# First layer of three experts by seven block products over even and odd tiles

## The reference

```python
def _moe_ref(x, domain_probs, w1, w2):          # x 1536x320, w1 4x320x1024, w2 4x1024x320
    p = domain_probs / (domain_probs.sum(-1, keepdims=True) + 1e-09)
    out = np.zeros((N, D), dtype=np.float32)
    for e in range(E):
        h = np.maximum(x @ w1[e], 0.0)
        out += p[:, e:e + 1] * (h @ w2[e])
    return out.astype(np.float32)
# the recurrence, for every token t:
#   C = f*C + i*outer(v, k);  n = f*n + i*k;  y = sigmoid(o) * (C @ q) / max(|n.q|, 1)
```

## Time and profile before

| what | value |
|---|---|
| median of 3 executions | 417.52 us |
| the profiled execution's own time | 416.59 us |
| its span, first to last instruction | 414.9 us |
| PE busy | 409.5 us (99%), 2698 matmuls |
| DVE, ACT, POOL busy | 180.0, 158.7, 147.4 us |
| granted TensorE clock | 0.999 of full speed |

### The profile page before, as it was taken

How to read it: one execution, slowest core, us unless ns; L and a number is a source line. 1 busy time by engine, 2 the same in 40 slices (tenths; PEclk the granted TensorE clock), 3 DMA queues, 4 the chain that set the end, 5 groups by cost and what they waited for, 6 DMA issues and landing times.

```text
span 414.9 us, 7006 instructions
## 1 busy us (share of the span) xinstructions
PE 409.5 (99%) x2698; PEld 396.1 (95%) x2698; DVE 180.0 (43%) x370; ACT 158.7 (38%) x329; POOL 147.4 (36%) x183
## 2 busy tenths in 40 slices
PE   8999999999999999999999999999999999999997
PEld 8889999999999999999999999999999999999996
DVE  6875796746555556446223232313123232311323
ACT  5475477745355643524122431234111342211111
POOL 5855735594175935302001650075100453000000
PEclk9999999999999999999999999999999999999999
DMA  8899939678513835300000331024200000000101
GB/s 276 268 294 377 355 106 362 233 261 284 190 43 118 311 124 206 125 2 0 2 0 2 92 125 63 0 71 140 71 0 0 2 0 2 34 0 0 65 0 65
DMA packets 16899, 48.45 MB, mean 117 GB/s; under 512 B 1921, under 2 KB 8594, under 8 KB 15714
## 3 DMA queue, kind: packets, MB, share of 16 engines
q1 hardware_dynamic: 16290, 46.60, 32.6%
q10 hardware_dynamic: 576, 1.40, 1.0%
HBM read 45.94 MB, written 2.05 MB: 116 GB/s over the span
## 4 chain that ended last, share of the span: by engine, by line
PE 96%; DVE 1%; ACT 1%; issue 1%; POOL 0%; DVEq 0%; POOLq 0%; ACTq 0%
PE hid_ps L1077 41%; PE acc_ps L1096 36%; PE out_ps L1033 5%; PE score_ps L1096 3%; PE out_ps L1040 2%; PE acc_ps L1077 2%; PE score_ps L977 2%; PE hid_ps L926 1%; PE add_ps L1012 1%; PE score_ps L972 1%; ACT dec_w L553 1%; PE acc_ps L1033 0%; PE out_ps L1052 0%; PE out_ps L1054 0%; PE out_ps L1053 0%
## 5 line engine op out<-in xcount | busy, mean ns | idle before, releaser
L811 DVE SCALAR_TENSOR_TENSOR h_lo<-hid_ps,h_hi 128x384 fp32r<-128x384 f32 (+2 forms) x120 | 68.0, 566 | 218.5 <-ACT h_hi L588 218.4
L588 ACT ACTIVATE h_hi<-hid_ps 128x384 fp32r<-128x384 f32 (+2 forms) x120 | 59.8, 498 | 230.7 <-PE hid_ps L1077 230.6
L1096 PE MATMUL acc_ps<-w_hi,h_hi 128*128 128x320 f32 x352 | 110.2, 313 | 0.0
L1096 PE MATMUL acc_ps<-w_hi,h_lo 128*128 128x320 f32 x352 | 108.8, 309 | 0.0
L1096 PE MATMUL acc_ps<-w_lo,h_hi 128*128 128x320 f32 x352 | 108.4, 308 | 0.0
L441 POOL TENSOR_TENSOR w_lo<-w_raw,w_hi 128x384 fp32r<-128x384 f32 x56 | 58.8, 1052 | 130.0 <-ACT w_hi L574 130.0
L1077 PE MATMUL hid_ps<-xt_hi,w_lo 128*128 128x384 f32 (+2 forms) x360 | 103.8, 342 | 0.6 <-POOL w_lo L441 0.6
L1077 PE MATMUL hid_ps<-xt_hi,w_hi 128*128 128x384 f32 (+2 forms) x360 | 104.2, 344 | 0.1
L1077 PEld LDWEIGHTS hid_ps<-xt_hi,w_lo 128*128 128x128 f32 x360 | 65.4, 188 | 5.0 <-POOL w_lo L441 0.8
L1096 PEld LDWEIGHTS acc_ps<-w_lo,h_hi 128*128 128x128 f32 x352 | 66.3, 188 | 1.3
L1096 PEld LDWEIGHTS acc_ps<-w_hi,h_hi 128*128 128x128 f32 x352 | 66.3, 188 | 1.3
...
## 6 DMA issues: line engine op xcount, KB each, us to landing
...
```

Of the source, the lines that this page charges most:

```text
L588: nc.scalar.activation(h_hi[:, M % RING, 0:cols], hid_bank(M)[:, 0:cols], ACT.Relu).then_inc(hid_hi, 1)
L811: nc.vector.scalar_tensor_tensor(h_lo[:, M % RING, 0:cols], hid_bank(M)[:, 0:cols], 0.0, h_hi[:, M % RING, 0:cols].bitcast(fp32), ALU.max, ...
L1096: last = nc.tensor.matmul(acc_ps[t][:, 0:DM], x, w, start=(f == 0 and i == 0), stop=(f == NF - 1 and i == 2))
```

## The change

Three experts on the later tiles are taken out of the slots: expert 2 on tiles 6 to 11, experts 1 and 0 on tiles 4 to 11. Ten groups (80 slots) are left, and expert 0 is loaded twice. The work taken out becomes 12 *steps*. A step takes two hidden blocks at a time and pairs of an even and an odd tile (3 pairs for expert 2, 4 pairs for the others). The first layer of a step is a product of a 2 x 2 block matrix of weights (2 hidden blocks by 2 halves of the 320 input rows, 160 each) and a 2 x 2 block matrix of `x` (2 halves of rows by even and odd tiles). It is computed with seven block products rather than eight, in the order 1, 6, 5, 7, 2, 4, 3. A product is 4 matmuls of pairs x 128 columns (128 rows high x high, low x high, high x low, and one over 96 rows with the three parts of the other 32).

The operands are sums. `t_hi`, `t_lo` and `rest` (sums and differences of `x`) are made once, in slots 64 to 72. For that, 24 DMAs copy 32-row pieces of `xt_hi` to other partitions (`load_rest`). The sums of the weights are made in each step: GpSimd makes the four sums (`step_sums`) and residuals (`own_lows`, `step_down_low`), ScalarE rounds (`own_highs`, `sums_highs`, `step_down_high`), VectorE makes residuals (`sums_lows`, `step_rest_low`). After the products VectorE, ScalarE and GpSimd combine them (`add_2`, `add_3`, `add_21`, `add_12`, `keep_1`, `keep_5`, `add_22`), then come ReLU and residual for each of the four blocks (`wide_relu`, `wide_low`). The second layer stays as it was: `wide_down`, 6 matmuls of 320 columns for one tile and two hidden blocks. The products of step 0 stand in slots 73 to 79, one at the end of each.

The core of the diff:

```diff
-LOADS = (0, 1, 2, 3, 2, 1, 0)
-GROUPS = ((0, 0, 2), (1, 0, 2), (1, 2, 2), (2, 0, 3), (2, 3, 3), (3, 0, 3), (3, 3, 3), (3, 6, 3), (3, 9, 3),
-          (4, 6, 3), (4, 9, 3), (5, 4, 4), (5, 8, 4), (6, 10, 2), (6, 2, 4), (6, 6, 4))
+LOADS = (0, 1, 0, 2, 3)
+GROUPS = ((0, 0, 2), (1, 0, 2), (1, 2, 2), (2, 2, 2), (3, 0, 3), (3, 3, 3), (4, 0, 3), (4, 3, 3), (4, 6, 3), (4, 9, 3))
-T0 = {2: 2, 3: 6, 4: 16, 5: 22, 6: 28, 7: 32, 8: 38, 9: 44, 10: 48, 11: 54}
+T0 = {2: 2, 3: 6, 4: 16, 5: 22, 6: 30, 7: 35, 8: 41, 9: 47, 10: 51, 11: 57}
+EXPERTS = (2, 1, 0)
+FIRST_PAIR = (1, 0, 0)
+ORDER = (1, 6, 5, 7, 2, 4, 3)
+BEGIN = 73
# SyncE
+            def load_rest():
+                wait_attention(sp)
+                for part, raised, lowered in ((rest_hi, 64, 96), (rest_lo, 0, 32)):
+                    for k, first in enumerate((raised, lowered)):
+                        source = halves(xt_hi[first:first + 32, 2, :].bitcast(fp32))
+                        for r in range(3):
+                            for half in range(2):
+                                to = part[32 * r:32 * (r + 1), (0, 3, 1, 2)[2 * k + half], :]
+                                sp.dma_start(to.rearrange(...), source[:, half, :, :]).then_inc(rest_in, 16)
...
+                if M == T0[NT - 1] + 7:
+                    load_rest()
# GpSimd
+            def rest_whole(first):
+                pool.wait_ge(rest_in, 24 * 16)
+                both = rest_hi[:, first:first + 2, :]
+                nc.gpsimd.tensor_tensor(both, both, rest_lo[:, first:first + 2, :], ALU.add).then_inc(rest_ready, 1)
...
+            for t in range(1, STEPS):
+                if t + 1 < STEPS:
+                    step_sums(t + 1)
+                    own_lows(t + 1)
+                    step_down_low(t + 1)
+                add_22(t)
# ScalarE, at the end of slots 68 and 71
+                if M == 68:
+                    round_rest(0, 3)          # waits for both rest_whole
...
+                if M == 71:
+                    round_rest(3, 2)          # waits for the four sums of turn_rest
+                    round_rest(5, 2)
# VectorE, a step
+            for t in range(1, STEPS):
+                add_wide(t, 0)
+                add_2(t)
+                add_wide(t, 1)
+                add_wide(t, 2)
+                add_3(t)
+                add_wide(t, 3)
+                if t + 1 < STEPS:
+                    sums_lows(t + 1)
+                wide_low(t, 11)
+                add_21(t)
+                if t + 1 < STEPS:
+                    step_rest_low(t + 1)
+                wide_low(t, 22)
+                wide_low(t, 21)
+                add_12(t)
+                wide_low(t, 12)
# TensorE
+                nc.tensor.matmul(to, hi[:, 0:128], x_hi, start=m in (1, 5, 6), stop=False, skip_group_check=True)
+                nc.tensor.matmul(to, lo, x_hi, start=False, stop=False, skip_group_check=True)
+                nc.tensor.matmul(to, hi[:, 0:128], x_lo, start=False, stop=False, skip_group_check=True)
+                nc.tensor.matmul(to, hi[0:REM, 128:256], rest[:, right, cols(t)], start=False, stop=True, ...)
...
+                if M >= BEGIN:
+                    product(0, ORDER[M - BEGIN])
+            for t in range(1, STEPS + 2):
+                ahead, behind = halves_of(t)
+                turns = [(half_of, i) for half_of in (ahead, behind) if half_of is not None for i in range(pairs(half_of[1]))]
+                for n in range(8):
+                    if t < STEPS and n < len(ORDER):
+                        product(t, ORDER[n])
+                    at = n if t > 1 else n - 1
+                    if 0 <= at < len(turns):
+                        wide_down(*turns[at][0], turns[at][1])
```

More of the change, by code:

```diff
@@ L123, with pair_of, pairs, downs_done @@
 LAST_GROUP = {n: max(a for a, g in enumerate(GROUPS) if g[1] <= n < g[1] + g[2]) for n in range(NT)}
+CLASSIC = EVICT[-1][0] + GROUPS[-1][2]
+def pair_of(t):
+    return FIRST_PAIR[2 * t // NF]
+def pairs(t):
+    return PAIRS - pair_of(t)
+def downs_done(t):
+    return sum(pairs(p) for p in range(t + 1))
+def wide_evictions(p, half, i):
+    before = [pairs(2 * b) for b in range(p // 2) for _ in range(2)] + [pairs(p)] * half
+    return CLASSIC + sum(before) + i + 1
+def last_evictions():
+    out = []
+    for pair in range(PAIRS):
+        p = max(p for p in range(1, STEPS, 2) if pair_of(p) <= pair)
+        out += [(wide_evictions(p, half, pair - pair_of(p)), FIRST_WIDE + 2 * pair + half) for half in range(2)]
+    return out
+def bank_freed(p, half, i):
+    if half == 1:
+        return wide_evictions(p, 0, i)
+    return wide_evictions(p - 2, 1, min(i, pairs(p - 2) - 1))
+def product_count(t, m):
+    return len(ORDER) * t + ORDER.index(m) + 1
+def halves_of(t):
+    first, second = ((0, t - 1), (1, t - 2)) if t % 2 == 0 else ((1, t - 2), (0, t - 1))
+    return [(half, p) if 0 <= p < STEPS else None for half, p in (first, second)]
 def wait_if(eng, sem, count):
@@ new lines, in build @@
+        x_nat = first("x_nat", [L, B, DM])
+        apart = raw[:, :, :, :, :].rearrange("p k t h l -> p k (t h l)")
+        attention.close()
+        t_hi, t_lo, rest = sb("t_hi", [128, 4, WIDE], f32r), sb("t_lo", [128, 4, WIDE], f32r), sb("rest", [REM, 7, WIDE], f32r)
+        left_hi, left_lo = sb("left_hi", [128, 2, 7, 256], f32r), sb("left_lo", [128, 2, 7, 128], f32r)
+        whole = between("whole", [128, 4, WIDE])
+        rest_hi, rest_lo = between("rest_hi", [REM, 4, WIDE]), between("rest_lo", [REM, 4, WIDE])
@@ L1195 @@
         "w_b": w.reshape(NE, NF // 2, 2, 128, WB).transpose(0, 1, 3, 2, 4),
+        "w_s": steps.reshape(STEPS, 128, SUM_AT),
     }
```

441 lines of the change are left out of this document (408 added, 33 removed).

## The result

| | before | after |
|---|---|---|
| time, median of 4 runs each (lowest to highest) | 417.39 us (416.86 to 417.92) | 429.14 us (427.77 to 430.61) |
| ratio | | 1.028, 95% interval 1.024 to 1.032 |
| profiled execution, time and span | 416.59, 414.9 | 430.01, 428.3 |

The change made the kernel 2.8% slower, 11.8 us between the medians. The forecast was slower too, but by 2.6 to 3 us, and 429 lies outside its range of 410 to 425.5.

A forecast was written before the change was run, and what follows sets the result against it. PE was taken as the bound, its time proportional to streamed columns plus waits. -10.1 + 5.9 + 7.2 = +3.0 us on 416.59 gave 419.6, or 420.5 by the median; forecast 420, range 410 to 425.5.

The forecast's parts named there:

- What it removes: On PE, 16 matmuls of 384 columns and 32 of 512 go: 10.1 us less.
- Slots 0 to 63: Before slot 64, same kind of work per slot on each engine: priced at nothing, 0 to 1 us.
- Part 1: Slots 64 to 73, operands from x: 24 DMA issues take 9.3 us; PE waits 1.7 us if nothing interferes.
- Part 2: Slots 67 to 73: VectorE and GpSimd exclude each other, raising PE's waits to 5.9 us instead of 1.7.
- a sign of being wrong: Forecast is wrong if L1279 and L1288 on VectorE keep to 0.65 and 1.07 us.
- Part 3: Steps 1 to 5: PE waits on VectorE's chains, 4.5 us without meeting GpSimd, 7.2 us with it.
- Part 4: Steps 6 to 11: VectorE needs 4.2 us against PE's 4.5, so nothing waits, by 0.3 us.
- rival (c): Steps 6 to 11 wait too, at each first wide_down on block 21's residual: 6 us more, 426; chance 0.12.
- the bound of 427: Upper end of the unknown: the longest VectorE and GpSimd operations in every encounter give about 427 us.

The follow-up runs named there:

- Experiment 5: Changed kernel with VectorE's two subtractions of unit 6's rounded scores in slots 25 and 26 in place of 26 and 28; 427.26 us, ratio 1.025.
- experiment 10: On top of experiment 9: the next step's own blocks rounded and their residuals formed earlier, tile-sum evictions ahead of x's gate in slots 39 and 55; 416.30 us, 0.996.
- experiment 8: Changed kernel with the 24 transfers of load_rest read from DRAM (rows of the weights) instead of xt_hi in SBUF; 426.71 us, ratio 1.023.
- Experiment 1: Changed kernel with 12 DMAs in load_rest instead of 24, each carrying both halves in the tiles' own order; 424.50 us, ratio 1.016.
- experiment 6: On top of Experiment 1 and Experiment 5: GpSimd forms one rest-row sum, VectorE the other and turn_rest's four subtractions, ScalarE's round_rest placed where its input is ready; 421.78 us.
- experiment 9: On top of experiment 6: VectorE forms both rest-row sums, GpSimd's step_sums(1) moves from slot 70 to 64, t_lows(0) and rest_lows(0, 3, 0) one slot later; 421.46 us.
- Experiment 11: Changed kernel with GpSimd's sums and residuals of the weights of steps 2 to 11 on 16, 8 and 32 columns only; 426.12 us, ratio 1.022.
- experiment 2: Changed kernel with 42 unused matmuls of 384 columns put ahead of block 70's second layer; 430.12 us, ratio 1.030.
- experiment 3: Changed kernel with DN_END 24 in place of 28, so GpSimd, not VectorE, takes the second-layer weight residuals of blocks 24 to 27; 430.78 us, ratio 1.031.
- experiment 4: Changed kernel with step_rest_low on one of seven weight blocks (128 columns in place of 896); 425.19 us, ratio 1.019.
- experiment 12: On top of experiment 10: step_rest_low(0), t_lows(0), rest_lows(0, 3, 0), own_highs(0) and sums_highs(0) in earlier slots, own_highs(1) one later; 411.75 us, ratio 0.986.

## Why the prediction was wrong

**What it removes: right.** -10.2 us measured for -10.1, and a step of seven products with four pairs takes 13.5 us where 13.4 was forecast. The 0.229 us per 512 columns of the earlier trace rows held after the change as well. The Trainium skill's 131 ns for them (TensorE: Matmul & The Clock Gate, section Back-to-back issue gap) did not show up here either.

**Slots 0 to 63: the first failed step.** "I price that at nothing" (0 to 1 us) measured +6.3 us. The argument was that each engine has the same kind of work per slot. It has, but in 2-tile slots, which are shorter, and with unit 6's subtractions at other slots relative to it. The order shows it: VectorE's second `subtract_high` of unit 6 now stands behind `xt_low(5)`, before the change it stood ahead of it, and the scores that need it fall in the slot without a block ahead. I had not followed this part of the order. Experiment 5 shows that this one place makes PE's wait of 2.1 us, and with it the low clock that can follow. The waits of 0.6 us at 135 and 192 us are two evictions that stand behind x's gate; in experiment 10, which puts them ahead of it, 0.3 us remain of each, before scores.

**Part 1, the issue of 24 transfers: the second failed step.** "Three take 1.16 us, so 24 take 9.3 us" measured 16.0. The earlier trace rows were transfers from DRAM; these read SBUF, and by experiment 8 that is 0.60 against 0.43 us an issue. It shifted the chain by 6.6 us, and 7.2 us of wait appeared in one piece before block 70 in place of 1. Experiment 1 takes the issue back to 8.8 us and gives 5.0 us of waits, with 5.9 forecast. Of the 9.9 us of the changed kernel 7.2 are this wait and 2.7 low clock. The other links (2.4, 1.5, 0.49 and 0.56 us) held to a tenth.

**Part 2, the meetings: right as a mechanism, absent in the changed kernel's own stretch.** Operations of 0.69 us took 2.8 beside GpSimd's in experiments 1 and 6, and 0.69 once it was idle (experiment 9). In the changed kernel GpSimd began only when VectorE had already run dry: `sums_lows` (L1279) took 0.69 and `step_rest_low` (L1288) 1.08 there, which the prediction had named as a sign of being wrong. The rule in the Trainium skill (SBUF — State Buffer, section "Who interferes with whom"), that a VectorE instruction with two SBUF inputs contends with a GpSimd instruction that reads SBUF, agrees with the 0.69 and the 2.8.

**Part 3, the steps: right in the main.** 7.1 us for 7.2, nearly all at the places named: 1.2 us in step 1 for block 21's residual (before product 6, not before the first `wide_down`), 1.6 before product 1 of step 2 with L1288 as releaser, 0.8 before its first `wide_down`, less in steps 3 to 5. Experiment 11 splits them as forecast: 4.5 us without GpSimd's work on the weights (4.5), 2.4 with it (2.7). **Part 4, steps 6 to 11: nearly right.** PE waits 0.7 us before the first `wide_down` of step 6, the place that rival (c) named, and nowhere from 340 us on.

**The clock** was in no term of the sum. In the changed kernel it was low behind the waits of 2.1 and 7.2 us. The wait alone does not decide it. Seven profiled executions have the wait at 97 us, those of the changed kernel and of experiments 1, 2, 3, 4, 8 and 11. In five of them the clock was low for 3.4 us behind it, in experiments 2 and 11 not at all. The windows of the changed kernel and of experiment 11, and experiment 11's wait:

```profile
99.00:103.00 4.00, 3.40 (x17) 3.43 (x18) 3.29 (x6) 1.91 (x6) 4.00 (x4) 0.75 0.49 176
99.00:103.00 4.00, 3.75 (x25) 3.78 (x26) 3.17 (x7) 2.30 (x6) 4.00 (x4) 1.00 0.59 200
99.25 0.63 PE L1483 MATMUL score_ps<-split_qk 128*128 128x128 f32 x4 [2.09 <-DVE split_qk L1110]
```

From 95 to 106 us PE lost 3.9 us against its stream with the low clock and 2.4 without it, so the low clock cost 1.5 us. Before block 70 it lay under a chain that would have held PE anyway: from 228 to 262 us PE lost 10.2 us with 10.2 us at the lower level, 10.4 us in experiment 11 with 6.8, and 10.4 us in experiment 2 with none (7.3 of them its useless matmuls). Executions of one kernel differ by it: the changed kernel's four had a mean clock of 0.984 at 430.0 and 430.6 us, and of 0.992 and 0.991 at 427.8 and 428.3.

**The rivals.** (c) named 426 as the far end, for steps 6 to 11, of which only step 6 waited, 0.7 us. No rival was for the stretch before slot 64, and the bound of 427 "in every encounter" left the price of the issue out, which rested on one row. A range with 0.39 to twice that for each of 24 issues would have reached 429.

**What stays open:** why the clock falls behind the same wait in one execution and not in another; the 1.1 us before 60 us, where small waits for weights come and go between kernels with the same code there (experiment 12's profiled execution, with such waits and a low clock behind them, was 3.7 us over its median); and what makes an issue in experiment 8 take 0.43 us where the carries take 0.37.
